# Attention, channel mix and gated convolution in one kernel: w_k tiles 4 to 7 of half 0 as split products, other cuts and warm-up

## The chip, the cores and the metric

The kernel runs on one core of a Trainium2 chip. The metric is device time in microseconds. A core has TensorE (matmuls into PSUM), VectorE, ScalarE and GpSimd (elementwise work) and SyncE, which here only issues transfers. The engines run their own instruction streams and wait for each other by semaphores. In the profile they are PE (PEld for its weight loads), DVE, ACT, POOL and SP; a q behind the name means that the engine issued a transfer.

## The reference, cut to what matters

Inputs are float32: q, k, v of 4 batches, 8 heads, 576 positions, head size 64. Heads 0 to 3 attend locally (the last 32 positions), heads 4 to 7 with stride 32.

```python
x = softmax(q k^T / 8 + mask) v            # 4 x 576 x 512, heads side by side
x_prev = x shifted by one position
xk = mu_k * x + (1 - mu_k) * x_prev
xr = mu_r * x + (1 - mu_r) * x_prev
x2 = sigmoid(xr @ w_r) * (relu(xk @ w_k)**2 @ w_v)   # w_k 512x1024, w_v 1024x512, w_r 512x512
h = relu(x2 @ w_in)                        # 512x1024
out = (h * sigmoid(conv3(h))) @ w_out      # conv of 3 taps along the positions; w_out 1024x512
```

## The kernel before

The first stage (attention and channel mix) works through eight halves of 288 positions, two for each batch. A second stage, the gated convolution, follows over whole batches and is not touched.

Matrix products come in two kinds. A plain product multiplies float32 operands as they are (`plain_product`). A split product (`product`) has each operand as a high part, rounded to the format fp32r, and a low part, the difference; it takes three matmuls for each of the four 128-row steps: high by high, high weight by low x, low weight by high x. In half 0 the w_k and w_r products are plain, since the weights have just arrived; in the other halves all are split, and the high and low parts of the weights are made meanwhile: w_k's high part on ScalarE (`high_w1`), its low part on GpSimd (`low_w1`).

Each half h goes through 20 slots. Slots 0 to 7 are the eight tiles of w_k (128 output columns each), 8 to 11 those of w_r, 12 to 19 the halves of the four w_v tiles. Into the slots the attention of half h + 1 is laid: tables `PLAN` and `SECOND` (the latter for half 1) say in which slot each block's scores, exponentials, normalizing and values come. Block 0 is local, block 1 strided. For half 1 the local scores are in slot 2, the strided ones in slot 5, the local values in slot 7, the strided ones in slot 11. Every engine walks through the same slots in its own program order; nothing is reordered at run time.

Around the change, on each engine:

- TensorE: warm-up matmuls on zeros (`keep_warm`), the attention of half 0, then the slots. `EARLY_M`, `EARLY_T` put the first two steps of tiles 0 to 3 ahead of the slots. In slots 1 and 3 it also turns half 1's q and k (`turn_rows`).
- VectorE: makes x_k (`mix_k`: a difference, then a scaled sum, into `xk_raw` in half 0), x_r (`mix_r`), copies turned k from PSUM (`lay_k`), masks and takes maxima (`mask_and_max`), normalizes and transposes (`normalize`), copies values out (`copy_out`), and makes the low part of x_k (`low_xk`) for halves 1 and up.
- ScalarE: exponentials, relu and square, high parts of x_k, x_r and w_k, copies of turned q (`lay_q`).
- GpSimd: low parts, of the squared activations (`low_k2`, k_lo in the profile) and of weights. The squared activations are in a ring of four buffers.
- SyncE: transfers in the order of its code. w_k's four of 512 KB, then v for half 0, rows of q and k, the other weights, v for half 1 (vl local, vs strided).

In half 7 the strided values are issued in two parts, in slots 12 and 13, and their copy comes one slot later than in the other halves.

Of the kernel before, what the change touches and what calls it, by code (L numbers as in the profile page):

```python
# [10 lines left out]
P = 128  # L11
# [5 lines left out]
def attention_channel_mix_gated_conv(  # L17
# [53 lines left out]

    RING = 3
# [4 lines left out]
    WARM_START, WARM_COLS, WARM_SLOT = 23, 224, 4  # L77

# [13 lines left out]
    with ExitStack() as ctx:  # L92
# [37 lines left out]

        OUT_BANKS = (2 * GRING, 2 * GRING + 1, 2 * GRING - 2, 2 * GRING - 1, 2 * GRING)
# [3 lines left out]
        diff = sb("diff", [P, KT, HALF], stack=mix)  # L135

        with ExitStack() as early:
            xk_raw = sb("xk_raw", [P, KT, HALF], stack=early)
            xr_raw = sb("xr_raw", [P, KT, HALF], stack=early)
        xk_hi, xr_hi, xk_lo, xr_lo = (  # L140
            sb(n, [P, KT, HALF], F32R, mix) for n in ("xk_hi", "xr_hi", "xk_lo", "xr_lo"))
# [11 lines left out]
        with ExitStack() as att:  # L153

            raw = sb("raw", [P, 2, 2 * PAIRS, JH, STRIDE], stack=att)
# [38 lines left out]
        wv_hi_dve, wv_lo_dve = sem("wv_hi_dve"), sem("wv_lo_dve")  # L194

# [120 lines left out]
        def load_raw(eng, b, c, strided, pairs):  # L316
            h = 2 * b + c

            wait(eng, turned, 4 * h if strided else 4 * h - 2)
            for T, src in enumerate((q, k)):  # L320
                for pair in pairs:
                    for x in range(2):
                        s = src[b, (HG if strided else 0) + 2 * pair + x]
                        s = s.rearrange("(j r) (y d) -> y r j d", r=STRIDE, y=2)
                        for y in range(2):
                            p0 = D * x + STRIDE * y
                            eng.dma_start(raw[p0:p0 + STRIDE, T, (PAIRS if strided else 0) + pair],
                                          s[y][:, JH * c:JH * c + JH]).then_inc(raw_loaded[strided], 16)
# [105 lines left out]
        def _(pool):  # L434
# [34 lines left out]
            def low_w1(i):  # L469

                _, raw_w, hi, lo = weights1[i]
                if i < WK_IN:
                    pool.wait_ge(w1_hi_act, WV_POOL + i + 1)
                    pool.wait_ge(tile_done, FT)
                elif i < WR_IN:
                    pool.wait_ge(w1_hi_dve, i - WK_IN + 1)
                    pool.wait_ge(tile_done, FT + KT)
                else:
                    pool.wait_ge(w1_hi_act, (i - WR_IN) // 2 + 1)

                n = LOW_COLS
                pieces = [(x, y) for x in range(hi.shape[1]) for y in range(0, hi.shape[2], n)]
# [11 lines left out]

            after = {4: (0,), 6: (2,)}
# [32 lines left out]
        def _(pe):  # L528
# [95 lines left out]
            def attention(h, slot):  # L624
                for i in of_slot(h, 3, slot):
                    if h == NH - 1 and blocks(h)[i][0] == STR:
                        values(h, i, 0)
                    else:
                        values(h, i)
                for i in of_slot(h, 3, slot - 1):  # L630
                    if h == NH - 1 and blocks(h)[i][0] == STR:
# [53 lines left out]
            def mlp(h, s):  # L685
# [8 lines left out]
                if h == 0 and s < FT:  # L694
                    plain_w_k(s, range(EARLY_T if s < EARLY_M else 0, KT)).then_inc(tile_done, 1)
                elif h == 0 and s < FT + KT:
# [6 lines left out]
                elif s < FT:  # L703
                    cols = slice(P * s, P * s + P)
                    product(bank,
                            lambda t: wa_hi[:, t, cols], lambda t: wa_lo[:, t, cols],
                            lambda t: xk_hi[:, t, :], lambda t: xk_lo[:, t, :],
                            xk_done if s == 0 else None, KT * h,
# [45 lines left out]
            keep_warm(WARM_SLOT + WARM_SLOT // 2)  # L754
# [74 lines left out]
        def _(act):  # L829
# [50 lines left out]
            def high_w1(i):  # L880
                _, raw_w, hi, _ = weights1[i]
                act.wait_ge(w1_loaded[i], 16)
                nc.scalar.copy(hi, raw_w).then_inc(w1_hi_act, 1)
# [4 lines left out]
            act.sem_inc(xk_hi_done, KT)  # L888
# [25 lines left out]
            exps(0, 2)  # L914

            act.wait_ge(o_done, block_at(1))
            for pair, which in ((0, 1), (1, 0), (1, 1)):
                src, dst = strided_out(0, (pair,), which)
                copied = nc.scalar.copy(dst, src)
                if which:  # L920
                    copied.then_inc(first_copied, 1)

# [76 lines left out]
        def _(dve):  # L999
# [74 lines left out]
            def attention(h, slot):  # L1074
                for i in of_slot(h, 3, slot):
                    if not (h == NH - 1 and blocks(h)[i][0] == STR):
                        copy_out(h, i)
                for i in of_slot(h, 3, slot - 1):
                    if h == NH - 1 and blocks(h)[i][0] == STR:
# [23 lines left out]
            def low_xk(h, t):  # L1103
                wait(dve, xk_hi_done, KT * h + t + 1)
                if t == 0:
                    wait(dve, tile_done, TILES * (h - 1) + FT)
                nc.vector.tensor_tensor(xk_lo[:, t], mixed[:, t], xk_hi[:, t].bitcast(F32),
                                        ALU.subtract).then_inc(xk_done, 1)

            def mix_r(h, t):  # L1110
# [3 lines left out]
                wait(dve, xk_done, KT * h + t + 1)  # L1114
# [42 lines left out]
            dve.sem_inc(xk_done, KT)  # L1157
# [52 lines left out]
            for h in range(NH):  # L1210
                ahead = h < NH - 1
                for slot in range(SLOTS):
# [4 lines left out]
                    if ahead:  # L1217
                        attention(h + 1, slot)
                    if slot == 0:
# [114 lines left out]
```

## Time and profile before

| | us |
|---|---|
| median of 3 runs (527.14 to 528.98) | 527.3 |
| profiled execution | 526.64 |
| its span, first to last instruction | 524.8 |
| TensorE busy (matmuls) | 516.7, 98% |
| VectorE busy | 322.5, 61% |
| ScalarE busy | 287.6, 55% |
| GpSimd busy | 114.7, 22% |

The span is what the profile shows; the run's time is 1.8 us longer, for what lies around the first and last instruction. A busy TensorE is one with a matmul in its pipeline: an instruction's duration includes its way through the array, so the pitch from start to start is what counts when many follow each other.

### The profile page before, as it was taken

To read this page: it belongs to the slowest core of one execution; us is meant where nothing else is said; L and a number is where in the kernel's file an instruction comes from. 1 tells how busy PE (TensorE), PEld (TensorE's weight loads), DVE (VectorE), ACT (ScalarE), POOL (GpSimd) and SP (SyncE) were. 2 spreads that over 40 slices of the span, in tenths; PEclk is the share of its full clock that TensorE was granted. 3 is DMA by queue.
4 is the path that set the end of the run, shared out by engine and by line. 5 is a ranking of instruction groups with operands and counts; after the bars stand their busy time and mean duration, and the time that the engine had idled before them with its cause. 6 is when DMAs were issued, how large, how long until landed. Compare 5 with 4: busy or idle time off the path is not lost.

```text
span 524.8 us, 15350 instructions
## 1 busy us (share of the span) xinstructions
PE 516.7 (98%) x6202; PEld 479.0 (91%) x6202; DVE 322.5 (61%) x812; ACT 287.6 (55%) x783; POOL 114.7 (22%) x139
## 2 busy tenths in 40 slices
PE   8799999999999999999999999999999999999997
PEld 6578999999999999999999999988998899889985
DVE  5769986657657566657644736881497049707910
ACT  4389288296394592691880815751583057416720
POOL 8039973031021040140221791000000000000000
PEclk9999999999999999999999999999999999999999
DMA  9893424343243332341106136001301130010011
GB/s 191 205 278 54 73 79 68 63 94 65 57 96 65 90 62 52 83 69 41 49 2 252 45 90 208 2 0 61 110 1 34 48 110 0 36 45 0 0 40 60
DMA packets 98772, 39.07 MB, mean 74 GB/s; under 512 B 91156, under 2 KB 91284, under 8 KB 98708
## 3 DMA queue, kind: packets, MB, share of 16 engines
q1 hardware_dynamic: 94334, 33.16, 25.6%
q0 software_dynamic: 1632, 4.36, 2.5%
q10 hardware_dynamic: 2742, 0.66, 0.8%
q8 instruction: 44, 0.72, 0.6%
q14 instruction: 20, 0.16, 0.1%
HBM read 28.72 MB, written 9.44 MB: 73 GB/s over the span
## 4 chain that ended last, share of the span: by engine, by line
PE 92%; SPq 6%; DMA 1%; issue 0%; ACT 0%
PE ps L788 19%; PE ps L798 19%; PE ps L680 9%; PE ps L681 9%; PE ps L682 8%; PE ps L731 7%; PE ps L732 7%; PE ps L733 6%; SPq L338 3%; PE ps L556 2%; PE ps L618 2%; PE ps L666 2%; SPq L350 2%; PE ps L599 1%; DMA vl<-in_v_dram 1%; SPq L383 1%
## 5 line engine op out<-in xcount | busy, mean ns | idle before, releaser
L492 POOL TENSOR_TENSOR k_lo<-k,k_hi 128x288 fp32r<-128x288 f32 x64 | 59.4, 931 | 192.6 <-ACT k_hi L860 192.5
L1275 DVE SCALAR_TENSOR_TENSOR cbuf<-hbuf,cols_c,cbuf 128x576 f32<-128x576 f32 x64 | 52.4, 819 | 63.5 <-ACT cbuf L965 62.4
L731 PE MATMUL ps<-k_hi,wb_hi 128*128 128x288 f32 x256 | 76.2, 298 | 0.0
L732 PE MATMUL ps<-k_lo,wb_hi 128*128 128x288 f32 x256 | 75.6, 295 | 0.0
L733 PE MATMUL ps<-k_hi,wb_lo 128*128 128x288 f32 x256 | 75.5, 295 | 0.0
L680 PE MATMUL ps<-xk_hi,wa_hi 128*128 128x288 f32 x224 | 67.1, 300 | 0.0
L681 PE MATMUL ps<-xk_lo,wa_hi 128*128 128x288 f32 x224 | 66.2, 295 | 0.0
L682 PE MATMUL ps<-xk_hi,wa_lo 128*128 128x288 f32 x224 | 66.1, 295 | 0.0
L798 PE MATMUL ps<-wb_hi,g_hi 128*128 128x512 f32 x144 | 57.5, 399 | 0.0
L798 PE MATMUL ps<-wb_hi,g_lo 128*128 128x512 f32 x144 | 56.8, 394 | 0.0
L798 PE MATMUL ps<-wb_lo,g_hi 128*128 128x512 f32 x144 | 56.5, 392 | 0.0
L788 PE MATMUL ps<-x_hi,wa_lo 128*128 128x288 f32 x256 | 55.0, 296 | 0.0
L788 PE MATMUL ps<-x_hi,wa_hi 128*128 128x288 f32 x256 | 55.0, 296 | 0.0
L788 PE MATMUL ps<-x_lo,wa_hi 128*128 128x288 f32 x256 | 54.4, 294 | 0.0
L837 ACT ACTIVATE sm<-sm,nb 128x64 f32<-128x64 f32 (+1 forms) x160 | 52.2, 328 | 0.5 <-DVE nb L1035 0.5
L731 PEld LDWEIGHTS ps<-k_hi,wb_hi 128*128 128x128 f32 x256 | 48.2, 188 | 0.3
L732 PEld LDWEIGHTS ps<-k_lo,wb_hi 128*128 128x128 f32 x256 | 48.2, 188 | 0.1
L733 PEld LDWEIGHTS ps<-k_hi,wb_lo 128*128 128x128 f32 x256 | 48.2, 188 | 0.0
L992 ACT COPY ob<-ps 128x512 f32<-128x512 f32 x18 | 10.6, 586 | 63.1 <-PE ps L798 62.9
L878 ACT CAST xr_hi<-mixed 128x288 fp32r<-128x288 f32 x28 | 11.4, 431 | 60.5 <-DVE mixed L1116 60.5
L680 PEld LDWEIGHTS ps<-xk_hi,wa_hi 128*128 128x128 f32 x224 | 42.2, 188 | 0.9
L682 PEld LDWEIGHTS ps<-xk_hi,wa_lo 128*128 128x128 f32 x224 | 42.2, 188 | 0.0
(110 smaller groups left out, 1160.5 us busy)
## 6 DMA issues: line engine op xcount, KB each, us to landing
x2d<-x2s SPq DMA_DIRECT2D x8, 576.0 KB, 3.1
x2raw<-x2d SPq DMA_DIRECT2D x4, 1152.0 KB, 5.2
out_dram<-ob SPq DMA_DIRECT2D x16, 256.0 KB, 2.0
raw<-in_q_dram SPq DMA_DIRECT2D x96, 36.0 KB, 1.9
raw<-in_k_dram SPq DMA_DIRECT2D x96, 36.0 KB, 1.9
wk_raw<-in_moe_w_k_dram SPq DMA_DIRECT2D x4, 512.0 KB, 9.2
wv_raw<-in_moe_w_v_dram SPq DMA_DIRECT2D x4, 512.0 KB, 5.9
ws<-in_moe_w_in_dram POOLq DMA_DIRECT2D x4, 512.0 KB, 7.2
```

The source lines that it names most:

```text
L338: eng.dma_start(rows[:, strided, T, i], src).then_inc(rows_loaded[c][strided][T], 16)
L492: nc.gpsimd.tensor_tensor(k2_lo[:, m], k2[:, m % K2RING], k2_hi[:, m].bitcast(F32), ALU.subtract).then_inc(k2_done, 1)
L680: nc.tensor.matmul(dst, w_hi(t), x_hi(t), start=(t == 0), stop=False)
L681: nc.tensor.matmul(dst, w_hi(t), x_lo(t), start=False, stop=False)
L682: mm = nc.tensor.matmul(dst, w_lo(t), x_hi(t), start=False, stop=(t == KT - 1))
L731: nc.tensor.matmul(dst, wb_hi[:, f, cols], k2_hi[:, f, :], start=(f == 0), stop=False)
L732: nc.tensor.matmul(dst, wb_hi[:, f, cols], k2_lo[:, f, :], start=False, stop=False)
L733: mm = nc.tensor.matmul(dst, wb_lo[:, f, cols], k2_hi[:, f, :], start=False, stop=(f == FT - 1))
L788: mm = nc.tensor.matmul(ps[:, 2 * (m % GRING) + c, 0:HALF], w[:, t, cols], x[:, c, t, :], start=(n == 0), stop=(n == 3 * KT - 1))
L798: mm = nc.tensor.matmul(ps[:, OUT_BANKS[t], :], g[:, f, toks], w[:, f, :], start=(f == 0 and n == 0), stop=(f == FT - 1 and n == 2))
L837: nc.scalar.activation(e, e, ACT.Exp, bias=nb[:, r, a:a + 1], scale=SCALE, accum_out=den[:, r, a:a + 1]).then_inc(exped, 1)
L1275: nc.vector.scalar_tensor_tensor(out=c, in0=h[:, o:o + S], scalar=conv[:, o, m:m + 1], in1=c, op0=ALU.mult, op1=ALU.add).then_inc(conv_ste ...
```

## The change

In half 0 the w_k tiles 4 to 7 become split products. For that, four things are made early: w_k's columns 512 to 1023 as high part (`high_right`, on ScalarE) and low part (GpSimd, ahead of its first k_lo, behind a wait for all of xk), x_k's high part (ScalarE) and low part (VectorE, in slot 2 behind the local maxima of half 1). Before tile 4 TensorE waits for GpSimd's four low parts, and at each of its steps for one low part of x_k. The late conversion of w_k handles the left columns alone. The buffers of `xk_raw` and `xk_hi` change places: `xk_raw` now lies where `raw` (q and k of later halves) will be, so SyncE waits for tile 4 and the low parts before half 2's local loads.

The two-part strided values move from half 7 to half 3 (`CUT`). The six warm-up matmuls of 512 columns before half 0's first values become 30 of 102.

```diff
+    CUT = (3,)
+    WARM_MORE, WARM_LESS = 30, 102
+        PLAIN_M = FT // 2
+        PLAIN = P * PLAIN_M
...
+            if h == 2 and not strided:
+                wait(eng, tile_done, PLAIN_M)
+                wait(eng, xk_done, KT)
...
                 if i < WK_IN:
+                    cols = PLAIN
                     pool.wait_ge(w1_hi_act, WV_POOL + i + 1)
-                    pool.wait_ge(tile_done, FT)
+                    pool.wait_ge(tile_done, PLAIN_M)
...
+            pool.wait_ge(k_mixed, KT)
+            for i in range(WK_IN):
+                _, raw_w, hi, lo = weights1[i]
+                pool.wait_ge(wk_right_hi, i + 1)
+                nc.gpsimd.tensor_tensor(lo[:, :, PLAIN:], raw_w[:, :, PLAIN:], hi[:, :, PLAIN:].bitcast(F32),
+                                        ALU.subtract).then_inc(wk_right_lo, 1)
             after = {4: (0,), 6: (2,)}
             for m in range(FT):
                 low_k2(0, m)
...
-                    if h == NH - 1 and blocks(h)[i][0] == STR:
+                    if h in CUT and blocks(h)[i][0] == STR:
                         values(h, i, 0)
...
-                if h == 0 and s < FT:
+                if h == 0 and s < PLAIN_M:
                     plain_w_k(s, range(EARLY_T if s < EARLY_M else 0, KT)).then_inc(tile_done, 1)
...
                     cols = slice(P * s, P * s + P)
+                    if h == 0 and s == PLAIN_M:
+                        pe.wait_ge(wk_right_lo, KT)
                     product(bank,
...
-                            xk_done if s == 0 else None, KT * h,
+                            xk_done if s == (0 if h else PLAIN_M) else None, KT * h,
...
-            keep_warm(WARM_SLOT + WARM_SLOT // 2)
+            keep_warm(WARM_MORE, WARM_LESS)
...
+            def high_right(i):
+                _, raw_w, hi, _ = weights1[i]
+                act.wait_ge(w1_loaded[i], 16)
+                nc.scalar.copy(hi[:, :, PLAIN:], raw_w[:, :, PLAIN:]).then_inc(wk_right_hi, 1)
...
             exps(0, 2)
+            high_right(0)
+            high_right(1)
...
+            high_right(2)
+            high_right(3)
+            for t in range(KT):
+                act.wait_ge(k_mixed, t + 1)
+                nc.scalar.copy(xk_hi[:, t], xk_raw[:, t]).then_inc(xk_hi_done, 1)
...
-                if t == 0:
+                if h and t == 0:
                     wait(dve, tile_done, TILES * (h - 1) + FT)
-                nc.vector.tensor_tensor(xk_lo[:, t], mixed[:, t], xk_hi[:, t].bitcast(F32),
+                nc.vector.tensor_tensor(xk_lo[:, t], mixed[:, t] if h else xk_raw[:, t], xk_hi[:, t].bitcast(F32),
                                         ALU.subtract).then_inc(xk_done, 1)
...
+                    if h == 0 and slot == SECOND[0][0]:
+                        for t in range(KT):
+                            low_xk(0, t)
```

VectorE's program order before, from the last of half 1's local maxima (sm, mx) in slot 2 to the normalizing in slot 5; kT_s is half 1's strided k:

```order
L1030 ISA sm,mx<-ps,mask 128x64
L1030 ISA mx 128x1
L1035 TENSOR_SCALAR nb<-mx 128x9 [waits maxed]
L1116 SCALAR_TENSOR_TENSOR xr_raw<-diff,cols_c,xT 128x288 [waits xk_done,diffed] x2
L1180 COPY kT_s<-ps 128x9x32 [waits rows_turned] x2
L1043 TENSOR_SCALAR den<-den 128x9 [waits exped]
```

The same place after the change:

```order
L1067 ISA sm,mx<-ps,mask 128x64
L1067 ISA mx 128x1
L1072 TENSOR_SCALAR nb<-mx 128x9 [waits maxed]
L1144 TENSOR_TENSOR xk_lo<-xk_raw,xk_hi 128x288 [waits xk_hi_done] x4
L1154 SCALAR_TENSOR_TENSOR xr_raw<-diff,cols_c,xT 128x288 [waits diffed] x2
L1217 COPY kT_s<-ps 128x9x32 [waits rows_turned] x2
L1080 TENSOR_SCALAR den<-den 128x9 [waits exped]
```

Four subtractions have come ahead of the two x_r sums and of the two k copies.

TensorE's program order before, tile 3's last steps, tile 4 and the strided scores of half 1 (slots 3 to 5):

```order
L666 MATMUL ps<-xk_raw,wk_raw 128x288 x2
L666 MATMUL ps<-xk_raw,wk_raw 128x288 [waits relu_done]
L666 MATMUL ps<-xk_raw,wk_raw 128x288 x3
L556 MATMUL ps<-kT_s,qT 32x64 [waits maxed,k_laid,q_laid]
L556 MATMUL ps<-kT_s,qT 32x64 x43
```

The same place after (the strided scores are the last two rows; one of the four steps is left out at the "..."):

```order
L689 MATMUL ps<-xk_raw,wk_raw 128x288 x2
L703 MATMUL ps<-xk_hi,wa_hi 128x288 [waits xk_done,wk_right_lo,relu_done]
L704 MATMUL ps<-xk_lo,wa_hi 128x288
L705 MATMUL ps<-xk_hi,wa_lo 128x288
L703 MATMUL ps<-xk_hi,wa_hi 128x288 [waits xk_done]
L704 MATMUL ps<-xk_lo,wa_hi 128x288
L705 MATMUL ps<-xk_hi,wa_lo 128x288
...
L579 MATMUL ps<-kT_s,qT 32x64 [waits maxed,k_laid,q_laid]
L579 MATMUL ps<-kT_s,qT 32x64 x43
```

Tile 4 has twelve instructions instead of four and waits for VectorE and GpSimd; the strided scores wait as before, for the k copies of the order above among others.

## Rows read from the trace of the kernel before

**Rows 1.** The page: granted clock in 40 slices, and the chain by engine.

```profile
PEclk9999999999999999999999999999999999999999
PE 92%; SPq 6%; DMA 1%; issue 0%; ACT 0%
```

**Rows 2.** TensorE's waits: who, for whom, us in total, times, longest.

```profile
PE ps L618 <- issue: 0.8, 1, 0.8
```

**Rows 3.** Timeline of TensorE: start us, us, instruction, count, idle before.

```profile
11.98 1.25 PE L739 MATMUL ps<-warm 128*128 128x512 bf16 x5
...
14.90 0.90 PE L599 MATMUL ps<-pt,vl 32*64 32x32 f32 x48 [0.64 <-DVE pt L1054]
...
21.61 1.26 PE L618 MATMUL ps<-pt,vs 27*64 27x27 f32 x88 [0.81 <-issue]
...
31.18 3.10 PE L666 MATMUL ps<-xk_raw,wk_raw 128*128 128x288 f32 x12
34.22 1.11 PE L556 MATMUL ps<-kT_s,qT 64*32 64x64 f32 x88
35.25 4.15 PE L666 MATMUL ps<-xk_raw,wk_raw 128*128 128x288 f32 x16
39.46 1.14 PE L599 MATMUL ps<-pt,vl 32*64 32x32 f32 x88
40.53 2.21 PE L666 MATMUL ps<-xk_raw,wk_raw 128*128 128x288 f32 x8
...
48.49 1.96 PE L618 MATMUL ps<-pt,vs 27*64 27x27 f32 x176
...
124.56 1.96 PE L618 MATMUL ps<-pt,vs 27*64 27x27 f32 x176
```

**Rows 4.** The chain of waits, 38 to 42 us: start us, us, what.

```profile
32.91 6.50 DMA vl<-in_v_dram
```

**Rows 5.** Timeline of TensorE: first and last of a split tile's twelve.

```profile
65.11 0.29 PE L680 MATMUL ps<-xk_hi,wa_hi 128*128 128x288 f32 x1
...
66.57 0.29 PE L682 MATMUL ps<-xk_hi,wa_lo 128*128 128x288 f32 x1
```

**Rows 6.** Timeline of VectorE.

```profile
24.81 0.52 DVE L1100 SCALAR_TENSOR_TENSOR xk_raw<-diff,cols_c,xT 128x288 f32<-128x288 f32 x1
...
30.63 0.95 DVE L1116 SCALAR_TENSOR_TENSOR xr_raw<-diff,cols_c,xT 128x288 f32<-128x288 f32 x2
31.50 1.19 DVE L1180 COPY kT_s<-ps 128x288 f32<-128x288 f32 x2
...
46.40 0.91 DVE L1054 STREAM_TRANSPOSE pt<-sm 128x704 f32<-128x704 f32 x1
...
52.45 1.64 DVE L1107 TENSOR_TENSOR xk_lo<-mixed,xk_hi 128x288 fp32r<-128x288 f32 x2
...
131.90 0.78 DVE L1107 TENSOR_TENSOR xk_lo<-mixed,xk_hi 128x288 fp32r<-128x288 f32 x2
...
139.45 0.46 DVE L1138 TENSOR_TENSOR x2s<-ps,rg 128x288 f32<-128x288 f32 x1 [1.51 <-PE ps L733]
```

**Rows 7.** Timeline of ScalarE.

```profile
22.91 0.89 ACT L919 COPY xT<-ps 128x126 f32<-128x126 f32 x3 [5.98 <-PE ps L618]
26.48 0.70 ACT L905 COPY qT<-ps 128x288 f32<-128x288 f32 x2 [2.68 <-PE ps L656]
...
38.26 1.04 ACT L883 CAST wb_hi<-wv_raw 128x1024 fp32r<-128x1024 f32 x1
```

**Rows 8.** The tile wk_raw: ns min/median/max, starts; its transfers' time to landing.

```profile
L484 POOL TENSOR_TENSOR wa_lo<-wk_raw,wa_hi x16: 734/951/1189, 52.1 to 64.8; 128x256 fp32r<-128x256 f32 x16
...
DMA to landing us min/median/max: 7.0/9.2/11.0
```

**Rows 9.** Timeline of SyncE's issues.

```profile
9.68 3.22 SPq L361 DMA_DIRECT2D vs<-in_v_dram  x6
```

**Rows 10.** Timeline of GpSimd.

```profile
28.52 0.80 POOL L492 TENSOR_TENSOR k_lo<-k,k_hi 128x288 fp32r<-128x288 f32 x1 [15.96 <-ACT k_hi L860]
```

More of the change, by code:

```diff
@@ L135, in attention_channel_mix_gated_conv @@
         diff = sb("diff", [P, KT, HALF], stack=mix)
+        xk_hi = sb("xk_hi", [P, KT, HALF], F32R, mix)
         with ExitStack() as early:
-            xk_raw = sb("xk_raw", [P, KT, HALF], stack=early)
             xr_raw = sb("xr_raw", [P, KT, HALF], stack=early)
-        xk_hi, xr_hi, xk_lo, xr_lo = (
-            sb(n, [P, KT, HALF], F32R, mix) for n in ("xk_hi", "xr_hi", "xk_lo", "xr_lo"))
+        xr_hi, xk_lo, xr_lo = (sb(n, [P, KT, HALF], F32R, mix) for n in ("xr_hi", "xk_lo", "xr_lo"))
         rt = sb("rt", [P, 2, HALF], stack=mix)
@@ L153, in attention_channel_mix_gated_conv @@
         with ExitStack() as att:
+            with ExitStack() as early:
+                xk_raw = sb("xk_raw", [P, KT, HALF], stack=early)
             raw = sb("raw", [P, 2, 2 * PAIRS, JH, STRIDE], stack=att)
@@ L194, in attention_channel_mix_gated_conv @@
         wv_hi_dve, wv_lo_dve = sem("wv_hi_dve"), sem("wv_lo_dve")
+        wk_right_hi, wk_right_lo = sem("wk_right_hi"), sem("wk_right_lo")
         raw_loaded = [sem(f"raw_loaded_{n}") for n in ("local", "strided")]
@@ L471, in low_w1 @@
                 _, raw_w, hi, lo = weights1[i]
+                cols = hi.shape[2]
                 if i < WK_IN:
+                    cols = PLAIN
                     pool.wait_ge(w1_hi_act, WV_POOL + i + 1)
-                    pool.wait_ge(tile_done, FT)
+                    pool.wait_ge(tile_done, PLAIN_M)
                 elif i < WR_IN:
@@ L481, in low_w1 @@
                 n = LOW_COLS
-                pieces = [(x, y) for x in range(hi.shape[1]) for y in range(0, hi.shape[2], n)]
+                pieces = [(x, y) for x in range(hi.shape[1]) for y in range(0, cols, n)]
                 for x, y in pieces:
@@ L630, in attention @@
                 for i in of_slot(h, 3, slot - 1):
-                    if h == NH - 1 and blocks(h)[i][0] == STR:
+                    if h in CUT and blocks(h)[i][0] == STR:
                         values(h, i, 1)
@@ L693, in mlp @@
                     bank = ps[:, t % 4, 0:HALF]
-                if h == 0 and s < FT:
+                if h == 0 and s < PLAIN_M:
                     plain_w_k(s, range(EARLY_T if s < EARLY_M else 0, KT)).then_inc(tile_done, 1)
-                elif h == 0 and s < FT + KT:
+                elif h == 0 and FT <= s < FT + KT:
                     n = s - FT
@@ L882, in high_w1 @@
                 act.wait_ge(w1_loaded[i], 16)
-                nc.scalar.copy(hi, raw_w).then_inc(w1_hi_act, 1)
+                cols = slice(0, PLAIN if i < WK_IN else DM)
+                nc.scalar.copy(hi[:, :, cols], raw_w[:, :, cols]).then_inc(w1_hi_act, 1)
+            def high_right(i):
+                _, raw_w, hi, _ = weights1[i]
+                act.wait_ge(w1_loaded[i], 16)
+                nc.scalar.copy(hi[:, :, PLAIN:], raw_w[:, :, PLAIN:]).then_inc(wk_right_hi, 1)
             act.sem_inc(h_done, FT)
             act.sem_inc(g_hi_done, FT)
-            act.sem_inc(xk_hi_done, KT)
             act.sem_inc(xr_hi_done, KT)
@@ L1075, in attention @@
                 for i in of_slot(h, 3, slot):
-                    if not (h == NH - 1 and blocks(h)[i][0] == STR):
+                    if not (h in CUT and blocks(h)[i][0] == STR):
                         copy_out(h, i)
                 for i in of_slot(h, 3, slot - 1):
-                    if h == NH - 1 and blocks(h)[i][0] == STR:
+                    if h in CUT and blocks(h)[i][0] == STR:
                         copy_out(h, i)
@@ L1113, in mix_r @@
                 wait(dve, diffed, KT * h + t + 1)
-                wait(dve, xk_done, KT * h + t + 1)
+                if h:
+                    wait(dve, xk_done, KT * h + t + 1)
                 into = mixed[:, t] if h else xr_raw[:, t]
@@ L1154, in _ @@
             dve.sem_inc(g_lo_done, FT)
-            dve.sem_inc(xk_done, KT)
             dve.sem_inc(xr_done, KT)
```

## The prediction

> **What bounds the kernel now.** I began with the page: the granted clock stands at its top digit (2.4 GHz) in all 40 slices, and TensorE makes 92% of the chain that ended last [rows 1]. Work moved between the other engines therefore counts only where TensorE stands still for it; otherwise only TensorE's own instructions count. The list of TensorE's waits says where it stands still: only before 25 us, and its longest unexplained wait, 0.8 us before the strided values of half 0, has no engine as releaser [rows 2]. The timeline of TensorE shows what to look for next [rows 3]: the order from the warm-up at 11.98 to the strided values of half 1 at 48.49, and which rows carry an idle time (in brackets).
>
> Two places there are held by transfers. At 21.61 the strided values of half 0 start after that unexplained wait [rows 2, 3]. What stands among their semaphores beside VectorE's is v's last head, which SP issues from 9.68 on [rows 9], behind w_k, whose transfers take up to 11.0 us to land; the last, issued in the half microsecond before, lands at about 20 [rows 8]. The second place is 39.46, the local values of half 1. The chain of waits goes there through a vl transfer issued at 32.91, landing 6.50 us later at 39.41 [rows 4]. The sixteen plain instructions before it start at 35.25 and end at 39.40 with their pipeline's tail; TensorE could have issued at about 39.25 and stood 0.2 us. So a gain made before 39.4 us cannot get past that place, and a delay beyond 0.2 us does.
>
> **The change, part by part.**
>
> Products. A plain w_k step is two instructions in the trace. Eight of them take 2.21 us and sixteen 4.15 [rows 3], a pitch of (4.15 - 2.21) / 8 = 0.243 and 1.94 us for a tile of eight. The twelve of a split tile start between 65.11 and 66.57 [rows 5]: 1.46 / 11 = 0.133, or 1.59 us. The saving is 0.35 us a tile, 1.4 us for tiles 4 to 7.
>
> ScalarE's casts. 1024 columns take 1.04 us [rows 7], so 512 cost 0.5 to 1.04. Two go into the 5.98 us of idle time before 22.91. The other two and four xk_hi casts (0.35 each: two q copies of 288 columns take 0.70) come after 22.91 + 0.89 = 23.80 and end between 26.2 and 27.3. The q copies behind them began at 26.48, after 2.68 us of idle time [rows 7]. I take 0.6 for a cast (the half of 1.04 and a little for its start), so 26.4: hidden; at worst half 1's first scores are 0.8 late. Without this idle time the eight casts would put 3.5 to 5 us of ScalarE ahead of those scores.
>
> GpSimd's subtractions. Four of 128x512 wait until xk is mixed, 24.81 + 0.52 = 25.33 [rows 6]. Nearest rows: 0.80 us for 288 columns [rows 10]; 0.73 least and 0.95 median for 256 [rows 8]. So 512 cost 1.3 to 1.9. I take 1.45 to 1.5, since VectorE mostly reads PSUM beside them until 30.6: done at 31.3. TensorE reaches tile 4 after four of the twelve instructions at 31.18, so at 32.2 [rows 3]. Hidden by 0.9 us; at 1.9 each they end at 32.9 and cost 0.7. The first k_lo, 28.52 before [rows 10], waits behind them until 31.3. Later GpSimd has eight pieces less of the sixteen at 52 to 65 us [rows 8] and ScalarE about 2 us less; TensorE waits for neither there, so that is worth nothing.
>
> VectorE is the dear part. Four xk_lo are put ahead of two mix_r (0.95 us, from 30.63) and two strided k copies (1.19 us, from 31.50, ending at 32.69) [rows 6], and TensorE waits for those copies before the strided scores at 34.22 [rows 3]. Two xk_lo take 0.78 us where GpSimd idles (131.90) and 1.64 beside GpSimd's pieces (52.45) [rows 6]. Four cost 1.6 to 3.3 us, and mix_r beside GpSimd may take 1.6 instead of 0.95, so the copies end between 34.3 and 36.7. GpSimd has its last w_k piece and then two waiting k_lo just then. I take the contended price for all but one of the four, 2.9 us, and 0.25 for a late mix_r: 35.8.
>
> A rule of the Trainium skill bears here (SBUF — State Buffer, Who interferes with whom): a GpSimd instruction and a VectorE one with two SBUF inputs exclude each other for the whole instruction. The trace agrees in kind, by 0.78 against 1.64 us. By that rule each piece of 512 columns would hold VectorE twice as long as the 256-column ones at 52 us did, the copies would end at about 36.1, and the sum would be +0.8 instead of the one below.
>
> TensorE then. Tile 4 waits step by step for xk_lo (done at about 31.4, 32.2, 33.0, 33.5) and ends near 34.0; its 0.35 us is lost. The strided scores start at 35.9 instead of 34.22, +1.7. Tiles 5 and 6 give back 0.7, and the stall of 0.2 at 39.46 is swallowed: the local values start at 40.25, +0.8. Their other input, VectorE's normalize behind the copies (about 2 us), is there by 37.9. Tile 7 gives back 0.35: **+0.45 us, rounded to +0.5**. What is late next is the strided values of half 1: their transpose ended at 46.40 + 0.91 = 47.31 [rows 6] and they began at 48.49 [rows 3]. VectorE's work between is nearly back to back and hands on most of its 3 us of delay less its own idle time, about 1.3 us: 48.6, against TensorE at 48.9. Covered by 0.3 us.
>
> Warm-up. Six instructions of 512 columns become thirty of 102. Five took 1.25 us [rows 3]; by columns thirty cost 1.3, at the split products' pitch of 0.133 they cost 4.0. They start at 11.98, and the values behind them wait for VectorE until 14.90 [rows 3]: 2.9 us are free. The upper end is 1.1 late, of which 0.8 vanishes in the wait before 21.61. I take zero, since 102 columns are nearer to the lower end; at worst +0.3.
>
> Cuts. Half 3's strided values were one block of 176 instructions, 1.96 us [rows 3]; they get a second start, and half 7 loses one: zero on TensorE. VectorE's copy comes one slot later, about 3 us. Half 3's last xk_lo ended at 132.7, and its products begin when half 2's last tile is gated, about 139.4 [rows 6]. Covered by 6.7 us; without that cover it would cost up to 3.
>
> SP's new wait (four tiles, xk_lo done, both by 34 us) stands in front of raw loads that come behind 24 vs transfers. Those follow the vl of 32.91; six took 3.22 us [rows 9], so the loads are after 40: nothing.
>
> The sum is made against the profiled execution, 526.64 us around a span of 524.8: 527.1. The median of runs, 527.3, is 0.7 above it, and the chip's other executions are what is predicted: **527.8 us**.
>
> **Rivals.**
> (a) The exchange as told, +0.1 to +1.3: 55%.
> (b) VectorE is hardly hindered, the copies end by 34.5. TensorE then comes to the local values before 39.41, the vl transfer holds it, and only tile 7 counts: -0.35, so 526.9. For it: xk_lo's price of 0.78; against: two k_lo ready to run beside it. 22%.
> (c) The strided values of half 1 wait too. With every upper price the copies end at 36.7, VectorE's transpose at about 49.6, and with q or GpSimd late as well, 50.5: +1.3 to +2.2, 528.6 to 529.5. 12%.
> (d) The change does all it says, as if no transfer held 39.46: -1.4 - 0.2, so 525.7. The vl issues on SP do not move, which speaks against. 3%.
> (e) The other side: the clock falls to 1.2 GHz. TensorE would newly stand for 1.7 us at 34 us, with small matmuls around. A stretch of 3 to 6 us at the lower level costs half of itself, 1.5 to 3 us, on top of +0.5: 529.3 to 530.8. It decides as soon as one slice of the page shows less than full clock. Against: before 15 us TensorE stands and has small matmuls for longer, and every slice is full [rows 1]. 8%.
>
> **Numbers.** A measurement of this kernel tells about 0.5% from nothing, that is 524.7 to 529.9. (a) to (d) lie inside and so does half of (e), with a little left for what I do not see: same 0.92, slower 0.06, faster 0.02. The range goes from just under (b), 526.6, into the upper part of (c), 529.2.
>
> **What would show it.** Right: tiles 4 to 7 of w_k at a pitch of 0.133; TensorE idle for 1 to 2 us before the strided scores, released by VectorE's kT_s; four xk_lo over 2.5 to 3.3 us; the 512-column pieces over by 32; local values at about 40.2 with no vl ahead of them. Idle before tile 4 released by GpSimd would show my price of its pieces wrong, local values at 39.4 behind vl would show (b), idle before 49 released by VectorE's transpose (c).

## The result, and the profile after

| | before | after |
|---|---|---|
| median of 9 runs each, us | 527.54 (527.12 to 528.98) | 529.95 (527.98 to 532.25) |
| profiled execution, us | 526.64 | 530.73 |
| its span | 524.8 | 528.9 |

The ratio is 1.0041, 95% interval 1.0021 to 1.0061: slower by 0.4%, which is 2.2 us by the ratio and 2.4 us by the medians. The forecast was 527.8 with a range of 526.6 to 529.2, so the time lies 0.75 us above the range. The profiled execution is 4.1 us of span longer than that of before.

The page of the changed kernel: the granted clock in 40 slices, two rows of its transfer queues and the chain by engine.

```profile
PEclk9899899999999999999999999999999999999999
q8 instruction: 44, 0.72, 0.6%
q14 instruction: 21, 0.17, 0.1%
PE 97%; DVE 1%; issue 1%; ACT 0%; POOL 0%; DVEq 0%; POOLq 0%
```

Where [rows 1] had full clock everywhere, slices 2 and 5 (13 to 26 and 53 to 66 us) now show less. The chain runs through TensorE even more than before (97% for 92%): no transfer holds it any longer. The queue named instruction becomes important below.

TensorE's waits in the changed kernel (who, for whom, us in total, times, longest):

```profile
PE ps L764 <- issue: 2.1, 1, 2.1
PE ps L641 <- issue: 2.0, 2, 1.8
...
PE ps L579 <- issue: 1.3, 1, 1.3
```

"Issue" means that the profile shows nothing that was waited for. Before there were two such waits, 0.8 us before half 0's strided values [rows 2] and 0.6 us inside the warm-up, which [rows 3] leave out:

```profile
13.87 0.39 PE L739 MATMUL ps<-warm 128*128 128x512 bf16 x1 [0.64 <-issue]
```

L764 is the warm-up, L641 the strided values, L579 scores. Only the third was forecast. The timeline of TensorE puts them in place (start us, us, instruction, count, idle before):

```profile
11.84 0.40 PE L764 MATMUL ps<-warm 128*128 128x102 bf16 x5
14.37 1.41 PE L764 MATMUL ps<-warm 128*128 128x102 bf16 x25 [2.14 <-issue]
...
34.33 0.29 PE L705 MATMUL ps<-xk_hi,wa_lo 128*128 128x288 f32 x1
35.94 0.79 PE L579 MATMUL ps<-kT_s,qT 64*32 64x64 f32 x59 [1.31 <-issue]
...
40.34 0.87 PE L622 MATMUL ps<-pt,vl 32*64 32x32 f32 x64
...
49.02 1.95 PE L641 MATMUL ps<-pt,vs 27*64 27x27 f32 x175
52.77 0.18 PE L641 MATMUL ps<-pt,vs 27*64 27x27 f32 x1 [1.81 <-issue]
52.88 3.90 PE L689 MATMUL ps<-xr_raw,wr_raw 128*128 128x288 f32 x8
56.40 0.51 PE L756 MATMUL ps<-k_hi,wb_hi 128*128 128x288 f32 x1
```

Up to 49.02 this is the forecast: the strided values of half 1 begin 0.53 us later than in [rows 3]. Then comes what was not in it. These 176 matmuls stop before the last of them, at about 50.8, and go on at 52.77, 2.0 us later; no semaphore is waited for inside this group. I call such a halt without a releaser a stand. Behind it the eight w_r products of 288 columns, 2.21 us in the kernel before, take 3.90. The windows of TensorE say why (busy us and instructions of each engine, then granted clock, share of the DMA engines, GB/s):

```profile
50.00:52.00 2.00, 0.96 (x98) 0.87 (x86) 1.96 (x3) 1.81 (x5) 2.00 (x4) 1.00 0.37 60
52.00:54.00 2.00, 1.23 (x4) 0.84 (x4) 1.96 (x4) 0.82 (x2) 2.00 (x3) 0.74 0.37 60
54.00:56.00 2.00, 2.00 (x6) 1.43 (x5) 2.00 (x4) 0.13 (x1) 2.00 (x3) 0.50 0.45 74
```

(In this view the numbers behind the stretch are its length, then PE, PEld, DVE, ACT and POOL.) After the stand the granted clock is 0.50, 1.2 GHz of 2.4, until about 56.4. The first w_v product starts at 56.40, and in the kernel before it was here:

```profile
50.38 2.21 PE L666 MATMUL ps<-xr_raw,wr_raw 128*128 128x288 f32 x8
52.21 0.51 PE L731 MATMUL ps<-k_hi,wb_hi 128*128 128x288 f32 x1
```

4.2 us = 0.5 from ahead of the strided values + 2.0 of stand + 1.7 of low clock, and that is the whole difference of the spans.

VectorE's rows in the changed kernel, for the prediction's dear part:

```profile
25.62 1.96 DVE L1154 SCALAR_TENSOR_TENSOR xr_raw<-diff,cols_c,xT 128x288 f32<-128x288 f32 x2
...
31.12 2.76 DVE L1144 TENSOR_TENSOR xk_lo<-xk_raw,xk_hi 128x288 fp32r<-128x288 f32 x4
33.80 0.94 DVE L1154 SCALAR_TENSOR_TENSOR xr_raw<-diff,cols_c,xT 128x288 f32<-128x288 f32 x2
34.66 1.17 DVE L1217 COPY kT_s<-ps 128x288 f32<-128x288 f32 x2
```

and GpSimd's pieces, four in 5.38 us, 1.34 each:

```profile
25.79 5.38 POOL L516 TENSOR_TENSOR wa_lo<-wk_raw,wa_hi 128x512 fp32r<-128x512 f32 x4 [13.23 <-DVE xk_raw L1137]
```

**What stands.** TensorE's matmuls and weight loads, taken together in order of their start and numbered, show a pattern. The unexplained stands of warm-up and strided values come back at the same number in another execution, whatever time it is there, and the numbers are a multiple of 256 apart. The packets of the queue called instruction have 0.72 MB / 44 = 16 KB, 64 bytes for each of 256. The table, worked out from the trace's records, gives each stand from the start of its last instruction to that of the next, the number of the latter, and the time from the start of the queue's last packet to TensorE's going on.

```
kernel                stand, us        number   number mod 256   packet to going on
before                12.85 -> 13.87    449     193              3.33
after                 12.03 -> 14.37    449     193              2.66
after                 50.75 -> 52.77   1985     193              2.36
after, once more      53.63 -> 55.79   1983     191              2.35
```

So the theory: TensorE's program comes in blocks of 256 instructions by that queue, and where TensorE has used up one block faster than the next one comes, it stands until it is there, some 2.5 us after its load began. The traces bear it out beyond these four rows: the queue has 44 packets in each of the 14 profiles. Given in order to the block ends 449, 705 and so on, one to one, they reach to 11457, and no block end of these 616 was passed sooner than 2.35 us after its own packet had begun, with a stand or without. The fastest way through a block is a run of tiny matmuls: a strided block of 176 has, with its weight loads, 352 instructions in 1.96 us. The edit that I priced at nothing, other numbers of instructions, moves the block ends: 24 more warm-up matmuls and 16 more products, each with its weight load, are 80 instructions ahead of half 1's strided values. (The last row's number is two lower; some records are missing from a trace.)

The rival theory: the exchange of plain for split products makes the loss, by way of VectorE (a wait that the profile can't name, or the fall of the clock that rival (e) of the prediction had), and the count is chance.

### The profile page after: what moved, and what is told of

Read it like the earlier page. It is cut to its first block, busy times and chain, and to the rows that moved or that the text cites. A ratio compares the mean times of both kernels' runs of the same rounds, so it can differ in the third digit from the quotient of the medians.

```text
span 528.9 us, 15435 instructions
## 1 busy us (share of the span) xinstructions
PE 518.1 (98%) x6242; PEld 482.5 (91%) x6242; DVE 324.6 (61%) x816; ACT 289.4 (55%) x791; POOL 113.8 (22%) x135
## 4 chain that ended last, share of the span: by engine, by line
PE 97%; DVE 1%; issue 1%; ACT 0%; POOL 0%; DVEq 0%; POOLq 0%
PE ps L813 19%; PE ps L823 19%; PE ps L703 9%; PE ps L704 9%; PE ps L705 9%; PE ps L756 7%; PE ps L757 6%; PE ps L758 6%; PE ps L689 3%; PE ps L579 3%; PE ps L641 2%; PE ps L622 2%; PE ps L764 1%; PE ps L679 1%; DVE xk_lo L1144 0%
## 5 line engine op out<-in xcount | busy, mean ns | idle before, releaser
L703 PE MATMUL ps<-xk_hi,wa_hi 128*128 128x288 f32 x240 | 72.3, 301 | 0.1
L704 PE MATMUL ps<-xk_lo,wa_hi 128*128 128x288 f32 x240 | 70.9, 295 | 0.0
L705 PE MATMUL ps<-xk_hi,wa_lo 128*128 128x288 f32 x240 | 70.8, 295 | 0.0
L703 PEld LDWEIGHTS ps<-xk_hi,wa_hi 128*128 128x128 f32 x240 | 45.2, 188 | 1.4 <-DVE xk_lo L1144 0.3
L704 PEld LDWEIGHTS ps<-xk_lo,wa_hi 128*128 128x128 f32 x240 | 45.2, 188 | 0.1
L705 PEld LDWEIGHTS ps<-xk_hi,wa_lo 128*128 128x128 f32 x240 | 45.2, 188 | 0.0
```

What stands on the lines that cost most here:

```text
L703: nc.tensor.matmul(dst, w_hi(t), x_hi(t), start=(t == 0), stop=False)
L704: nc.tensor.matmul(dst, w_hi(t), x_lo(t), start=False, stop=False)
L705: mm = nc.tensor.matmul(dst, w_lo(t), x_hi(t), start=False, stop=(t == KT - 1))
```

## The experiments

Each ratio is against the kernel before on the same chip. The experiments ran on several chips, where the kernel before had 527.3 to 527.5 us; where two of them are compared, the difference is that of the medians, with that of the ratios beside it.

**The old warm-up.** The changed kernel, with six matmuls of 512 again.

```diff
-            keep_warm(WARM_MORE, WARM_LESS)
+            keep_warm(WARM_SLOT + WARM_SLOT // 2)
```

> The changed kernel with the old six warm-up matmuls of 512 columns: 24 matmuls and 24 weight loads fewer ahead of everything. Theory I (instruction blocks): TensorE's program comes in blocks of 16 KB, and in the changed kernel one whole block lies inside the 176 tiny strided-value matmuls of half 1 and is used up in 1.3 us, faster than the next arrives; that is the 2.0 us stand at 50.75 and the clock fall behind it. 48 instructions fewer move the block's end beyond the tiny matmuls, so no stand there, no clock fall at 53, and 528.0 us (the exchange on VectorE alone, +0.5 on 527.5). Theory II (the warm-up has nothing to do with it; the stand is a late v transfer of half 1 that the split products provoke): the stand stays and the time stays at about 530.

Measured: 530.84 (528.17 to 532.73), ratio 1.0063 [1.0043, 1.0084]. The stand at 50 us is gone, as expected, but the time is not better: 528.0 was forecast. Its timeline of TensorE has a new stand in another place, in the strided values of half 7, which the change issues in one part again:

```profile
273.18 1.70 PE L641 MATMUL ps<-pt,vs 27*64 27x27 f32 x150
276.73 0.47 PE L641 MATMUL ps<-pt,vs 27*64 27x27 f32 x26 [1.85 <-issue]
```

Its number is 9409, again 193 mod 256. A miss, since I had looked at the block end of half 1 alone; the mechanism stands better than before.

**The new warm-up alone.** The kernel before, with thirty of 102.

```diff
-            keep_warm(WARM_SLOT + WARM_SLOT // 2)
+            keep_warm(30, 102)
```

> The kernel before with thirty warm-up matmuls of 102 columns in place of six of 512, nothing else. Theory I: the block's end falls behind the tiny matmuls, no stand at 49 to 51; at the start the stand inside the warm-up comes after its fifth short matmul, is 2.1 us instead of 0.6 and the clock falls at about 15, most of it hidden by the transfer that holds 21.6: 527.6 to 528.2. Theory II (stand caused by the split products): 527.5. Were the new warm-up the whole of the loss: 530.

Measured: 528.55 (525.98 to 529.91), ratio 1.0015 [0.9998, 1.0032], a little above the range; the interval just includes nothing. The stand is at 449, before the sixth warm-up matmul, and 3.6 us long in this execution:

```profile
12.41 0.40 PE L739 MATMUL ps<-warm 128*128 128x102 bf16 x5
16.25 1.97 PE L739 MATMUL ps<-warm 128*128 128x102 bf16 x25 [3.45 <-issue]
```

In both kinds of warm-up it comes behind five matmuls. With six of 512 columns one is left to do after it, with thirty of 102 twenty-five are, and so half 0's values began at 15.71 in the changed kernel and at 14.90 in the one before; its first w_k products behind the strided values were 0.38 late (23.18 for 22.80). The stand is there in the kernel before as well (13.87 in its timeline), only shorter.

**80 instructions more, and nothing else.** The kernel before; its very first warm-up has 63 matmuls of 82 columns instead of 23 of 224, with about as many columns in all.

```diff
-    WARM_START, WARM_COLS, WARM_SLOT = 23, 224, 4
+    WARM_START, WARM_COLS, WARM_SLOT = 63, 82, 4
```

> The kernel before with its first warm-up as 63 matmuls of 82 columns instead of 23 of 224 (5166 columns for 5152): same columns, 80 more instructions on TensorE, as many as the changed kernel has more ahead of half 1's strided values. Theory I: a stand of about 2 us in those values near 50 us, the clock falls behind it in most executions, 530 to 531. Theory II: nothing at 50, 527.5.

Measured: 537.96 (536.95 to 538.66), ratio 1.0188 [1.0162, 1.0214], the largest effect of the study and far above the 530 to 531 forecast, with not one product, cast or copy changed. TensorE's timeline:

```profile
11.01 0.66 PE L556 MATMUL ps<-kT_s,qT 64*32 64x32 f32 x54 [0.26 <-DVE kT_s L1180]
15.08 0.51 PE L556 MATMUL ps<-kT_s,qT 64*32 64x32 f32 x34 [3.41 <-issue]
...
19.78 0.80 PE L599 MATMUL ps<-pt,vl 32*64 32x32 f32 x38 [0.26 <-DVE pt L1054]
23.46 0.47 PE L599 MATMUL ps<-pt,vl 32*64 32x64 f32 x2 [2.88 <-issue]
...
55.95 1.96 PE L618 MATMUL ps<-pt,vs 27*64 27x27 f32 x176
60.05 2.29 PE L666 MATMUL ps<-xr_raw,wr_raw 128*128 128x288 f32 x4 [2.14 <-issue]
```

Stands of 3.6, 3.1 and 2.3 us at 449, 705 and 1985, ended 2.4 to 2.6 us after a packet's start. The last is at the same place in half 1 as in the changed kernel, without the exchange: the rival can't have that. The first two, which I had not foreseen, fall into scores and values of half 0, on which everything behind waits: half 1's local scores start at 35.71 us, in the kernel before at 28.12. The granted clock stood at 0.50 behind all three, for 3.4, 6.8 and 3.4 us.

**Half 7 cut again.** The changed kernel, with its new warm-up.

```diff
-    CUT = (3,)
+    CUT = (7,)
```

> The changed kernel with the two-part strided values back in half 7 instead of half 3. Both theories: the place of the cut is worth nothing, 529.9 to 530. If the cut of half 7 mattered, the time would fall by more than 0.5 and TensorE would show idle time behind 250 us in the changed kernel.

Measured: 530.43 (529.89 to 532.01), ratio 1.0054 [1.0035, 1.0073]. The stand at 1985 is there (50.89 to 53.05, the clock at 0.50 in 54 to 56 us), none later: where the cut sits is not what costs in the changed kernel. That is close. With half 7 in one part, as in the changed kernel, block end 9409 lies in its strided values too; TensorE passed it 2.42 us after its packet and did not stand.

**The products alone.** The changed kernel, with both other edits undone: the old warm-up and half 7 cut.

> The changed kernel with the old warm-up and with the two-part strided values back in half 7: the split products and what they need, alone. Theory I (a block of 16 KB of TensorE's program inside a run of tiny matmuls is used up before the next has arrived): neither at 51 (the old warm-up moved it) nor at 275 (the cut in half 7 interrupts it) a stand; TensorE stands 1.5 us before the strided scores at 36, and the time is 527.6 to 528.1, +0.2 to +0.7 on the kernel before. Theory III (the products themselves make the clock fall, wherever it may be): a slice below full clock and 529.5 or more.

Measured: 527.81 (526.99 to 529.39), ratio 0.9999 [0.9986, 1.0012]. This differs from the first experiment by the cut alone and is 3.0 us faster (3.4 by the ratios), and from the fourth by the warm-up alone and is 2.6 us faster (2.9 by the ratios). Of TensorE's timeline:

```profile
16.59 0.39 PE L764 MATMUL ps<-warm 128*128 128x512 bf16 x1 [2.65 <-issue]
...
30.08 0.97 PE L579 MATMUL ps<-kT_l,qT 64*32 64x64 f32 x72
37.53 0.69 PE L579 MATMUL ps<-kT_s,qT 64*32 64x64 f32 x48 [1.31 <-issue]
41.93 1.14 PE L622 MATMUL ps<-pt,vl 32*64 32x32 f32 x88
```

The idle time of the exchange is here, 1.31 us, in full. What it costs in the times is 0.3 us by the medians and nothing by the ratio. The stand of 449 was 3.0 us in this execution; I come back to that.

**The products, with x_r's last two sums later.** As the one before, but VectorE makes `mix_r(0, 2)` and `mix_r(0, 3)` of half 0 behind the strided k copies.

```diff
+                        mix_r(0, 2)
+                        mix_r(0, 3)
...
-                        mix_r(h, 2)
-                        mix_r(h, 3)
+                        if h:
+                            mix_r(h, 2)
+                            mix_r(h, 3)
```

> As the products alone, and VectorE makes x_r's steps 2 and 3 of half 0 behind half 1's strided k copies instead of ahead of them. By the reading of the trace the copies end 0.94 us earlier, the strided scores start at about 35.0, and the local values of half 1 wait for nothing but the vl transfer that lands at about 39.4: 0.5 to 0.8 us faster than the products alone, 527.0 to 527.3. If the scores wait for something else than VectorE, it changes nothing.

Measured: 528.32 (526.72 to 529.37), ratio 1.0003 [0.9989, 1.0017]. In the trace it works:

```profile
30.24 0.97 PE L579 MATMUL ps<-kT_l,qT 64*32 64x64 f32 x72
36.85 1.09 PE L579 MATMUL ps<-kT_s,qT 64*32 64x64 f32 x88 [0.49 <-issue]
41.28 1.13 PE L622 MATMUL ps<-pt,vl 32*64 32x32 f32 x88
```

From the local scores of half 1 to its local values it is 11.04 us instead of 11.85, so 0.8 is won there. In the times it isn't seen, and 527.0 to 527.3 was forecast: a miss. The runs scatter by 2.7 us, more than the gain. In this one profile it is lost later: from the local scores to the first w_v product 0.4 us is left (23.82 for 24.25), and behind that product the span is 0.6 longer (473.3 for 472.8).

**Half 1 cut too.** The changed kernel with both other edits in, and a slow tile between the two parts of half 1's strided values.

```diff
-    CUT = (3,)
+    CUT = (1, 3)
```

> The changed kernel with half 1's strided values in two parts as well, so that the last w_r tile of 1.9 us stands between them. The count of instructions stays. Theory I: the block that was used up in 1.3 us now takes over 3 us, the 2.0 us stand at 50.8 and the clock fall behind it are gone; the new warm-up's own stand at 12 us stays: 528.0 to 528.6. Theory IV (the number of instructions or the warm-up as such costs the time): 530 as before.

Measured: 528.41 (526.8 to 529.96), ratio 1.0008 [0.9994, 1.0022], 1.5 us better than the changed kernel (1.7 by the ratios), with the same instructions in the same number. TensorE's timeline:

```profile
51.17 1.16 PE L641 MATMUL ps<-pt,vs 27*64 27x27 f32 x96
52.26 2.21 PE L689 MATMUL ps<-xr_raw,wr_raw 128*128 128x288 f32 x8
54.40 1.10 PE L641 MATMUL ps<-pt,vs 27*64 27x27 f32 x80
```

No stand in half 1. The eight slow products give the block 2 us more, and the next one is there, only just: the block end, now inside the second part, was passed 2.56 us after its packet. This is the sharpest test: the block ends stay where they are, and only the speed through the block is changed.

**The other cut alone.** The kernel before, with half 3 in two parts instead of half 7 (four conditions, the first shown).

```diff
-                    if h == NH - 1 and blocks(h)[i][0] == STR:
+                    if h == 3 and blocks(h)[i][0] == STR:
```

> The kernel before with the two-part strided values in half 3 instead of half 7, nothing else. I forecast zero for this. Theory I now: a block of the program lies wholly inside half 7's uninterrupted strided values (it starts 79 instructions into them), so TensorE stands about 1.8 us at 274, and the clock falls behind it in most executions: 529.5 to 531. By the forecast: 527.4.

Measured: 531.85 (529.02 to 533.63), ratio 1.0063 [1.0039, 1.0087]. TensorE's timeline at half 7:

```profile
274.30 1.83 PE L618 MATMUL ps<-pt,vs 27*64 27x27 f32 x167
278.47 0.35 PE L618 MATMUL ps<-pt,vs 27*64 27x27 f32 x9 [2.34 <-issue]
...
279.14 0.44 PE L733 MATMUL ps<-k_hi,wb_lo 128*128 128x288 f32 x1
279.38 0.44 PE L731 MATMUL ps<-k_hi,wb_hi 128*128 128x288 f32 x1
```

A stand of 2.5 us at 9409, the number of the first experiment's, and behind it products at a pitch of 0.24 us, half the clock, until 282.3. So half 7's cut in the kernel before keeps a block end from being met at speed: taking it out costs 4.3 us by the medians, 3.3 by the ratio (2.1 to 4.6). Read from [rows 3], a move of the cut looked like work of the same length in another place.

**All odd halves cut,** with the products (as in the sixth) and in the kernel before.

```diff
-    CUT = (7,)
+    CUT = (1, 3, 5, 7)
```

> Split products with the old warm-up, x_r's late steps behind the k copies, and the strided values of all odd halves (1, 3, 5, 7) in two parts, so that no block of TensorE's program can lie inside a run of tiny matmuls, whatever the count of instructions. Theory I: no stand behind 25 us but the one of about 0.5 us before the strided scores; 527.0 to 527.9, not clearly apart from the kernel before. A gain of more than 1 us would say that half 1, 3 or 5 lost time unseen in the kernel before as well.

> The kernel before with all odd halves cut in two parts. Theory I: no block stood still behind 25 us before and none does now: the same time within 0.2%. If a cut costs by itself (an output copied one slot later), the time rises by more than 0.5 us.

Measured: 528.28 (527.33 to 528.75), ratio 1.0012 [1.0, 1.0024], with the products; 529.58 (527.71 to 530.58), ratio 1.0026 [1.0011, 1.004], in the kernel before. The first has the smallest scatter of all kernels here, 1.4 us, but isn't faster and lies above its range of 527.0 to 527.9. The second is a miss: no stand behind 25 us, full clock, and yet 1.4 us by the ratio and 2.2 by the medians. I had written that this would show a cut to cost by itself, and the timelines say how much. From half 1's first w_v product to half 3's it is 73.86 us in the kernel before (89.02 to 162.88) and 74.26 in the eighth experiment, where half 3 is cut; from half 5's to half 7's it is 69.68 in the kernel before, with its cut, and 69.27 in the changed kernel without. So a cut costs TensorE 0.4 us, and three more of them cost 1.2. The trace also has a longer wait for ScalarE's `rt`, 0.47 us at 84.76, behind half 1's values, and a vl transfer that came later (0.91 us of idle time before 40.32):

```profile
40.32 1.14 PE L599 MATMUL ps<-pt,vl 32*64 32x32 f32 x88 [0.91 <-DMA vl<-in_v_dram]
...
84.76 0.40 PE L680 MATMUL ps<-xr_hi,wr_hi 128*128 128x288 f32 x1 [0.47 <-ACT rt L852]
```

The next profile of the kernel before has 0.23 us at that vl place and its local values 0.55 us earlier (39.77), so cuts and transfer make most of the 1.9 us between the spans (527.5 and 525.6). The late transfer stands ahead of the first cut; what made it late stays open.

**Both kernels once more,** one profile each.

> The kernel before, unchanged, profiled once more. Its first profile had a stand of 0.6 us inside the warm-up and no clock fall. If that stand is the load of a block against busy transfers, its length is chance: between 0.6 and 4 us in another execution, at the same instruction, with a clock fall behind it where it is long, and little of it in the time.

> The changed kernel, unchanged, profiled once more. Theory I: the stand of about 2 us inside the last matmuls of half 1's strided values is there again, at the same instruction, since it hangs on the program and not on chance; the stand at the start has another length.

Measured: 527.49 (span 525.6, clock 1.0) and 532.03 (span 530.2). TensorE's timeline of the second:

```profile
12.55 0.40 PE L764 MATMUL ps<-warm 128*128 128x102 bf16 x5
17.18 2.31 PE L764 MATMUL ps<-warm 128*128 128x102 bf16 x25 [4.23 <-issue]
...
51.90 1.95 PE L641 MATMUL ps<-pt,vs 27*64 27x27 f32 x175
55.79 0.18 PE L641 MATMUL ps<-pt,vs 27*64 27x27 f32 x1 [1.94 <-issue]
55.90 2.21 PE L689 MATMUL ps<-xr_raw,wr_raw 128*128 128x288 f32 x8
```

The kernel before has its stand at 449 again, 1.3 us long, and no fall of the clock. In the changed kernel the strided values begin 2.9 us later than in its first profile, and yet the stand comes behind the same 175 matmuls and is 2.1 us long (1.94 of them idle). It goes with the instruction, not with the time. Two things differ: the stand of the start is 4.2 instead of 2.1 us, and the clock does not fall at 56 (2.21 us for the eight products), where it fell in the first.

## Why the prediction was wrong

**What held.** The dear part was read well. The four xk_lo took 2.76 us, said 2.9; the k copies ended at 34.66 + 1.17 = 35.8, said 35.8; the strided scores started at 35.94, said 35.9; the local values at 40.34, said 40.25; the strided values of half 1 at 49.02, said 48.9. A part of this agreement is luck: everything was 0.38 us late already when half 1 began, from the start of the kernel, where the forecast had zero. Counted from half 1's local scores (28.12 before, 28.50 after), the exchange made the strided scores 1.34 us late for the 1.7 forecast, the local values 0.50 for 0.8 and the strided values 0.15 for 0.45: two of the four xk_lo paid for GpSimd beside them, not three, and the x_r sums behind them did not. Tile 4's saving was lost and those of tiles 5 and 6 given back, at the pitch of 0.133. The 512-column pieces took 1.34 us, a little under the 1.45 to 1.5 taken, and ended at 31.2 (31.3). The casts were hidden: q's copies began at 26.86, 0.38 later than before, as everything was at that point. SP's wait cost nothing. The products alone came out at 527.81, +0.3 by the medians and nothing by the ratio, where the sum said +0.5: the low side of rival (a).

The rule on the shared port (the Trainium skill, SBUF — State Buffer, Who interferes with whom) has better evidence now: VectorE's pair of x_r sums took 1.96 us beside the 512-column pieces and 0.94 at 33.80, where GpSimd was idle. The 36.1 for the copies, worked out from it, did not come: the 512-column pieces were over at 31.2, and what ran beside the first xk_lo were two k_lo of 288 columns.

**What failed** is one term of the sum, a zero: "Warm-up ... I take zero", at worst +0.3. As work it is nearly right. As a number of instructions it is not: the prediction counted what instructions take and never what they move in the program. The warm-up's 48 instructions, with the 32 of the products, put a block end where half 1's 352 fast instructions are: +2.6 us (the fourth against the fifth experiment), of which 2.0 are the stand. The whole change is 2.1 us slower than its products alone (529.95 against 527.81; 2.2 by the ratios). Breaking that one run of tiny matmuls takes 1.5 of it back (the seventh), and would take back more if the cut itself were free; the rest, 0.6 us, is within the intervals.

"Cuts ... zero on TensorE" came out right in the changed kernel, but by luck. As work it holds: half 3's new cut costs 0.4 us and half 7's, taken out, gives 0.4 back. But one part less in half 7 opens a second place for a stand, which costs where a block end is met at speed: +3.0 (the first against the fifth), +4.3 in the kernel before (the eighth; 3.3 by the ratio). In the changed kernel the block ends happen to lie so that only half 1 is hit.

**The clock** was rival (e), with the wrong trigger. I let it fall by TensorE's idle 1.3 us at 34 us; there it stayed full. It fell behind the 2.0 us at 50.8, behind that in half 7 (0.44 us for products that otherwise take 0.29), and at the start: in the ten profiles whose stand at 449 was 2.2 us or longer it fell behind it, in the four with 1.3 us or less it did not. So (e)'s time, 529.3 to 530.8, came true by another stall, which is luck for (e). It is not certain either: behind the same stand in half 1 it fell in the first profile and in the fourth experiment, and not in the last. The price of such a stand is thus 2.0 to 2.5 us, and up to 1.7 more; the medians, 2.1 to 4.3, agree with that. Of the changed kernel's nine executions, the two with a mean granted clock of 0.999 and 1.000 took 528.4 and 528.0 us and the seven with 0.992 to 0.997 took 529.6 to 532.3; whether the low clock or a longer stand with it makes that difference, times alone don't tell.

**The rows that could have told.** The kernel before has an idle time without a releaser at the start (0.64 us before 13.87), and the list of waits had "issue" as a name. I used the list to find which transfer it was. A run of short instructions before such a stand and the same place in each execution would have been the sign.

**What is not settled.** That the queue called instruction brings TensorE's program is inferred from the packets' size, their pace (one for each 256 of TensorE's numbers) and the delay to its going on; no view names the engine, and for the last four block ends, behind 11457, the queue shows no packets at all. The stand of the start, at 449, is 0.9 to 4.4 us long in the profiled kernels; what sets its length I didn't find. It is likely to make much of the scatter (1.0 us in the profile of before, 4.4 in the last one) and is partly hidden, since the values behind it wait for VectorE until 14.9. And a block end in other halves' strided values does not always cost: at 198.5 us in the kernel before TensorE entered a block that it was through in 1.26 us and did not stand; there the next load had begun 1.3 us ahead of the entry, and in the changed kernel's block of 49.5 us it began 0.9 us behind it. The traces show a part of why. Of the 602 loads in the 14 profiles, the first of each left out, none began sooner than 0.87 us after TensorE had started the instruction 56 ahead of the block before it, and half of them came within 1.5 us of that. Where a block begins 18 instructions into the tiny matmuls, as at 198.5, those 56 reach back into slow products, and the load begins early; where it begins 95 into them, as at 49.5, they take 0.3 us. TensorE was through these 56 and the block in 1.5 to 2.4 us at the six stands in halves 1 and 7, and in 3.8 us or more at 198.5 and in the seventh experiment, where it did not stand. Why some loads begin later than this least time stays open.

## What to carry to other kernels

Count instructions, not only time: an edit that costs nothing but changes how many instructions stand ahead of a run of several hundred tiny matmuls can cost or save 2 to 4 us, and an idle time of "issue" inside a group of instructions that waits for nothing, at the same instruction in each execution, is the sign. Before a cut, a padding or a warm-up count is judged, look where in TensorE's numbering the fast runs lie, and break with a slow tile the one that is met (half 1's cut took 1.5 us back with the same number of instructions). Break no others: each cut costs 0.4 us by itself. Judge an edit by itself: here the products alone cost nothing measurable, and a small edit that came with them, the warm-up, made the loss.

## What the runs showed of the hardware that was not expected

- TensorE stood at instructions 449, 705, 1985 and 9409 of its matmuls and weight loads (193 mod 256, but for one to three missing records), for 2.0 to 4.4 us, in the changed kernel (both profiles) and the first nine experiments, and went on 2.4 to 3.0 us after the last 16 KB packet of the instruction queue had begun.
- In 14 profiles no block end of 616 was passed sooner than 2.35 us after its own packet had begun.
- 80 instructions more in the first warm-up, with about the same columns, made the kernel 1.9% slower (537.96 us).
- Behind a stand of 2.0 to 2.5 us the granted clock went to 0.50 for about 3.4 us in some executions and stayed at 1.00 in another (the last run) at the same instruction.
